# Who issues the stores and weight loads of a Fourier stage: from ScalarE to SP, with two small changes of order

## The reference

```
X = np.fft.rfft(x, axis=1)                       # x: 2 x 3008 x 256
y = np.fft.irfft(X * (filt_r + 1j * filt_i)[None], n=3008, axis=1)
x = y.reshape(6016, 256)
h = x @ w_in;  x = elu(h) @ w_out                # first layer, 256 -> 2048 -> 256
h = x @ w_in2; out = (h * clip(h + 3, 0, 6) / 6) @ w_out2
```

## Time and profile before

| | |
|---|---|
| time, median of 3 | 1148.3 us (1145.12 to 1150.12) |
| time of the profiled execution | 1148.3 us |
| its span | 1145.6 us |
| PE, PEld busy | 1124.9, 1070.5 us |
| DVE, ACT, POOL busy | 850.8, 699.6, 305.0 us |
| Fourier stage | 0 to about 134 us |

### The profile page before, as it was taken

How to read it: one execution, slowest core, us unless ns; L and a number is a source line. 1 busy time by engine, 2 the same in 40 slices (tenths; PEclk the granted TensorE clock), 3 DMA queues, 4 the chain that set the end, 5 groups by cost and what they waited for, 6 DMA issues and landing times.

```text
span 1145.6 us, 17167 instructions
## 1 busy us (share of the span) xinstructions
PE 1124.9 (98%) x6280; PEld 1070.5 (93%) x6280; DVE 850.8 (74%) x1347; ACT 699.6 (61%) x1293; POOL 305.0 (27%) x260
## 2 busy tenths in 40 slices
PE   8999899999999999999998999999999999999998
PEld 4666799999999999999997899999999999999998
DVE  6777388788888888888888876666666666666665
ACT  0222466766666666666666666667666666766665
POOL 4876212030202112121248742120302021121000
PEclk9999999999999999999999999999999999999999
DMA  8886300000000101010021201000000000010000
GB/s 254 270 253 213 102 1 28 29 27 28 28 28 16 39 1 55 1 55 1 28 82 57 91 1 54 1 28 28 27 29 27 28 24 32 1 55 1 28 1 27
DMA packets 33587, 59.50 MB, mean 52 GB/s; under 512 B 3456, under 2 KB 23552, under 8 KB 33504
## 3 DMA queue, kind: packets, MB, share of 16 engines
q1 hardware_dynamic: 27168, 48.06, 13.4%
q10 hardware_dynamic: 6336, 10.36, 2.7%
HBM read 39.92 MB, written 18.48 MB: 51 GB/s over the span
## 4 chain that ended last, share of the span: by engine, by line
PE 91%; DVE 4%; ACT 1%; DMA 1%; issue 1%; POOL 1%; SPq 0%; ACTq 0%
PE ps L360 43%; PE ps L349 13%; PE ps L350 13%; PE ps L351 13%; PE ps L292 2%; PE ps L317 2%; PE ps L308 2%; PE ps L309 2%; DVE e L584 2%; PE ps L300 2%; DVE e L582 1%; DVE g_lo L589 1%; DMA x_ring<-x_dev 1%; ACT e L465 1%; ACT w_hi L442 0%
## 5 line engine op out<-in xcount | busy, mean ns | idle before, releaser
L589 DVE TENSOR_TENSOR g_lo<-e,g_hi 128x376 fp32r<-128x376 f32 (+1 forms) x384 | 285.6, 771 | 113.6 <-ACT g_hi L495 113.3
L349 PE MATMUL ps<-op_hi,w_hi 128*128 128x376 f32 x896 | 300.3, 335 | 0.7 <-DVE h L603 0.7
L350 PE MATMUL ps<-op_hi,w_lo 128*128 128x376 f32 x896 | 299.7, 334 | 0.0
L351 PE MATMUL ps<-op_lo,w_hi 128*128 128x376 f32 x896 | 299.6, 334 | 0.0
L654 POOL TENSOR_TENSOR op_lo<-xr,op_hi 128x752 fp32r<-128x752 f32 x64 | 103.9, 1624 | 623.6 <-ACT op_hi L450 623.6
L360 PE MATMUL ps<-g_hi,w_hi 128*128 128x376 f32 x1024 | 259.1, 334 | 7.3 <-ACT g_hi L495 7.3
L360 PE MATMUL ps<-g_lo,w_hi 128*128 128x376 f32 x1024 | 259.5, 335 | 2.0 <-DVE g_lo L589 1.9
L360 PE MATMUL ps<-g_hi,w_lo 128*128 128x376 f32 x1024 | 259.6, 334 | 0.0
L360 PEld LDWEIGHTS ps<-g_hi,w_hi 128*128 128x128 f32 x1024 | 184.0, 188 | 9.4 <-ACT g_hi L495 9.4
L360 PEld LDWEIGHTS ps<-g_lo,w_hi 128*128 128x128 f32 x1024 | 184.1, 188 | 5.0 <-DVE g_lo L589 5.0
L360 PEld LDWEIGHTS ps<-g_hi,w_lo 128*128 128x128 f32 x1024 | 184.2, 188 | 0.0
(11 more groups left out here) (50 smaller groups left out, 1216.6 us busy)
## 6 DMA issues: line engine op xcount, KB each, us to landing
f_ring<-f_dev SPq DMA_DIRECT2D x32, 384.0 KB, 4.4
xr<-y SPq DMA_DIRECT2D x64, 188.0 KB, 3.0
y<-ystage SPq DMA_DIRECT2D x16, 376.0 KB, 2.5
out_dev<-ystage SPq DMA_DIRECT2D x16, 376.0 KB, 2.5
x_ring<-x_dev SPq DMA_DIRECT2D x15, 384.0 KB, 5.5
y<-ystage ACTq DMA_DIRECT2D x24, 235.0 KB, 2.8
w_raw<-w_dev ACTq DMA_DIRECT2D x16, 256.0 KB, 4.5
w_raw<-w_dev SPq DMA_DIRECT2D x16, 256.0 KB, 2.8
```

The costliest lines, as they stand in the source:

```text
L349: pe.matmul(out, w_hi[:, p, cols], hi, start=start, stop=False, skip_group_check=True)
L350: pe.matmul(out, w_lo[:, p, cols], hi, start=False, stop=False, skip_group_check=True)
L351: pe.matmul(out, w_hi[:, p, cols], lo, start=False, stop=True, skip_group_check=True).then_inc(done, 1)
L589: return dve.tensor_tensor(g_lo[:, tiles, :], e[:, tiles, :], f32(g_hi[:, tiles, :]), ALU.subtract)
```

## The change

SP gets store_piece and all of load_w. In each step it runs load_f, load_x, the store of piece_at(i-1) and, in step w_step(p) - 2, load_w(p); load_w(0) stands behind the first x and filter loads instead of ahead of everything on ScalarE's queue. The last store stands behind the loop, ahead of load_xr(1). On ScalarE the cast weight_hi(p) now stands ahead of the evacuation of its step. The matmul engine runs six warm-up matmuls instead of two. The condition `and i` that goes away changes nothing (at i = 0 the first comparison is false already). The sizes, the slots, the waits and the work of PE, DVE and POOL in each step stay.

```diff
--- before.py
+++ after.py
@@ -219,12 +219,21 @@
                 sp.dma_start(f_ring[:, i % FSLOTS].rearrange("p a n -> p (a n)"),
                              f_dev[c // B, :, g]).then_inc(f_loaded[i % FSLOTS], 16)
 
+            def store_piece(n):
+                pos, j0, nj = piece_cols(n)
+                c = ORDER[pos]
+                at = c % B * S + j0 * ICOL
+                sp.wait_ge(i_evac, n + 1)
+                sp.dma_start(y0[c // B, :, at:at + nj * ICOL],
+                             ystage[:, n % 2, 0:nj * ICOL]).then_inc(y0_stored[n % 2], 16)
+
             def load_w(k):
-                p = k % PAIRS
-                sp.wait_ge(w_lo_done, k - 1)
+                layer, p = k // PAIRS, k % PAIRS
+                if k >= 2:
+                    sp.wait_ge(w_lo_done, k - 1)
                 raw = w_raw[:, k % 2]
-                sp.dma_start(raw[:, 0:4 * P], w_dev[1, p, :, 0:4 * P]).then_inc(w_loaded[k % 2], 16)
-                sp.dma_start(raw[:, 8 * P:12 * P], w_dev[1, p, :, 4 * P:8 * P]).then_inc(w_loaded[k % 2], 16)
+                sp.dma_start(raw[:, 0:4 * P], w_dev[layer, p, :, 0:4 * P]).then_inc(w_loaded[k % 2], 16)
+                sp.dma_start(raw[:, 8 * P:12 * P], w_dev[layer, p, :, 4 * P:8 * P]).then_inc(w_loaded[k % 2], 16)
 
             def load_xr(s):
                 if s:
@@ -258,13 +267,21 @@
             load_f(2)
             load_x(2)
             load_x(3)
+            load_w(0)
             for i in range(NG + PIECES):
-                if FSLOTS <= i + FSLOTS - 1 < NG and i:
+                if FSLOTS <= i + FSLOTS - 1 < NG:
                     load_f(i + FSLOTS - 1)
                 if i % 2 == 0 and XSLOTS <= i // 2 + 3 < NG // 2:
                     load_x(i // 2 + 3)
+                done = piece_at(i - 1)
+                if done is not None:
+                    store_piece(done)
+                for p in range(1, PAIRS):
+                    if i == w_step(p) - 2:
+                        load_w(p)
                 if i == 26:
                     load_xr(0)
+            store_piece(NPIECE - 1)
             for s in range(2 * NS):
                 if s + 1 < 2 * NS:
                     load_xr(s + 1)
@@ -319,7 +336,7 @@
                 last.then_inc(i_done, 1)
 
             pe.wait_ge(zeroed, 1)
-            for _ in range(2):
+            for _ in range(6):
                 pe.matmul(ps[:, 0, :], back[:, 0, 0, :], back[:, 0, 0:4, :].rearrange("p j d -> p (j d)"),
                           start=True, stop=True)
             pe.wait_ge(a_mat_loaded, 16)
@@ -411,28 +428,12 @@
 
         @block.scalar
         def _(act):
-            def store_piece(n):
-                pos, j0, nj = piece_cols(n)
-                c = ORDER[pos]
-                at = c % B * S + j0 * ICOL
-                act.wait_ge(i_evac, n + 1)
-                act.dma_start(y0[c // B, :, at:at + nj * ICOL],
-                             ystage[:, n % 2, 0:nj * ICOL]).then_inc(y0_stored[n % 2], 16)
-
-            def load_w(p):
-                if p >= 2:
-                    act.wait_ge(w_lo_done, p - 1)
-                raw = w_raw[:, p % 2]
-                act.dma_start(raw[:, 0:4 * P], w_dev[0, p, :, 0:4 * P]).then_inc(w_loaded[p % 2], 16)
-                act.dma_start(raw[:, 8 * P:12 * P], w_dev[0, p, :, 4 * P:8 * P]).then_inc(w_loaded[p % 2], 16)
-
             def evac_piece(n):
                 nj = piece_cols(n)[2]
                 act.wait_ge(i_done, n + 1)
                 if n >= 2:
                     act.wait_ge(y0_stored[n % 2], 16 * (n // 2))
                 act.copy(ystage[:, n % 2, 0:nj * ICOL], ps_i(n)[:, 0:nj * ICOL]).then_inc(i_evac, 1)
-                store_piece(n)
 
             def weight_hi(k):
                 p = k % PAIRS
@@ -467,14 +468,12 @@
                     act.activation(dst, src, ACT.Relu, bias=3.0).then_inc(ready, 1)
 
             for i in range(NG + PIECES):
+                for p in range(PAIRS):
+                    if i == w_step(p):
+                        weight_hi(p)
                 n = piece_at(i - 1) if i <= NG else None
                 if n is not None:
                     evac_piece(n)
-                for p in range(PAIRS):
-                    if i == w_step(p) - 2:
-                        load_w(p)
-                    if i == w_step(p):
-                        weight_hi(p)
                 if NG <= i:
                     evac_piece(NPIECE - PIECES + i - NG)
                 if NG - NOP <= i < NG:
```

## The result

The changed kernel takes 1158.26 us (median of 5; 1157.18 to 1158.92) against 1148.9 for the kernel before in the same measurement: a ratio of 1.0084 (95% interval 1.0063 to 1.0103), 9.4 us slower. The forecast was the same 9.4 us, counted from the 1148.3 us of the first three timings: 1157.7 us. Executions of one kernel spread over some 5 us, and part of that is the clock: of the 89 timings of the kernel before that stand beside the experiments, the 21 with a mean granted clock of 1.000 took 1144.7 us on average and the other 68 took 1147.3. The profiled execution of the changed kernel took 1156.32 us with a span of 1154.5, so between the two profiled spans there are 8.9 us to explain.

The account below looks back on a forecast made before the run. The matmul engine, busy 98% of the span, was taken to bound the kernel. Ring 10.9, tail -1.5 and start 0 gave +9.4 on 1148.3, so 1157.7 us, with an 8-in-10 range of 1150.5 to 1164.

Parts of the forecast that it names:

- The ring: Fourier stage: evacuation, store, filter load, sign, sums, cast, back to evacuation; 13.7 us per turn against 11.1, delay 10.9 us.
- four lumps of 2 to 3 us: Fourier stage, 50 to 110 us: idle matmul time, one lump per weight pair, behind DVE's prod_i.
- the formula 5 L: Fourier stage: delay is 5 L - 9.6, L being a filter load from issue to landing, taken as 4.1 us.
- The fixed part of a turn: Fourier stage: one turn without its filter load (store issue, signs, weight_lo, sums, cast, evacuation), put at 9.6 us.
- Entry: Fourier stage, first turn: piece 2's evacuation ends at 50.3 us instead of 46.86.
- the exit: End of the Fourier stage's turns: piece 13 evacuated at 104.9, prod_i(26) at 110.4 instead of 99.52, 10.9 us late.
- The tail: Last output pieces of the Fourier stage: 1.5 us gained; up to 2.0 from the wait, 1.7 more from the clock.
- load_xr(1): Load now behind the last store, some 20 us later: costs nothing, covered by its first ScalarE reader at 159.0.
- The start: Six warm-up matmuls and later first weights at the kernel's beginning: taken as 0 us, ends -0.5 and +1.5.
- rival 1: Fourier stage: unseen slack with filter loads under 3.4 us, so no change within 0.5%; chance 0.20.
- Rival 2: Faster through the last output pieces, 3.7 us off, plus 1.0 at the beginning: 1143.6 us; chance 0.04.
- Rival 3: Fourier stage: clock falls after each turn's 2.6 us idle, at most 6.8 us on top, about 1164 us; chance 0.10.

Follow-up runs that it names:

- 1: The changed kernel with the evacuation ahead of weight_hi again on ScalarE, stores and weight loads still on SP: 1145.84 us, ratio 0.9993 to the kernel before.
- 4: The changed kernel, cast still first, with each store on SP put behind the next step's filter load: 1146.22 us, ratio 0.9999 to the kernel before.
- 2: The kernel before with weight_hi ahead of the evacuation and its store, all stores and weight loads still on ScalarE: 1146.37 us, ratio 1.0003.
- 3: The kernel before with only the stores of y0 moved to SP, the last one behind the loop: 1145.14 us, ratio 0.9987.
- 5: The changed kernel with one more 128x704 subtraction on POOL in weight_lo of pairs 3 to 7: 1164.48 us, ratio 1.0162 to the kernel before.
- 6: The kernel before with one more 128x704 subtraction on POOL in weight_lo of pairs 3 to 7: 1145.25 us, ratio 1.0001.
- experiment 10: The kernel before with six warm-up matmuls instead of two: 1147.93 us, ratio 1.0004.
- 9: The kernel before with one more wait on SP, holding load_xr(1) until the last evacuation, stores still on ScalarE: 1146.3 us, ratio 0.9994.
- 11: The kernel before with only the first layer's weight loads moved to SP, stores on ScalarE, evacuation first: 1147.74 us, ratio 1.0012.

## Why the prediction was right, point by point

**The ring** is shown: its chain stands in the profile, its cost goes away with either of two unlike edits (1 opens it, 4 makes it shorter than PE's own time), it does not exist with either half alone (2 and 3), and work added inside it comes out nearly one for one (5) but is free outside (6). The likeliest case and its mechanism held. One thing stays open. No run has only the cast first and the stores on SP, so what the weight loads on SP and the warm-up add to the ring isn't shown; its chain runs through no weight load after 50 us. And one thing the forecast had only in part: it put all of PE's waits behind prod_i, in four lumps of 2 to 3 us; there were six of up to 1.6 us, and two of them were part_i's own wait for an evacuation, which the forecast didn't name. Both ways end in the same ring, so its length, and not the way, set the time.

**The size of the ring's term** was met (10.9 forecast, 10.4 measured) partly by luck: its errors cancel. The filter load took 4.36 to 4.86 us, 4.63 on average, not 4.1: by the formula 5 L, 2.7 us too little. The fixed part of a turn was 9.3 us (13.67 - 4.36, and 9.29, 9.32, 9.36 for the others), not 9.6: 1.1 too much over four turns. Entry: piece 2's evacuation ended at 50.67, forecast 50.3. So prod_i(26) came at 112.37, 12.9 us late, not 10.9. Then the exit was wrong in kind: I let the ring end with piece 13, but weight_lo(7) still stands ahead of group 27's sign in POOL's program, and prod_i(27) came at 116.60 (103.43 before, in its timeline), 13.2 us late. For PE this exit is worth only 0.3 us: part_r(26) was 10.2 us late, part_r(27) 10.5. And I took DVE's lateness for PE's, which is the largest of the errors beside that of the filter load. In the kernel before, prod_i(27) ended at 103.98 and its first reader, part_r(27), started at 106.67: 2.7 us of slack that the delay uses up first. 13.2 - 2.7 is 10.5.

**The tail** gained 3.3 us where 1.5 was taken. About 2 us are the shorter wait (7.9 us instead of 10.0 between pieces 21 and 27), as bounded by 2.0. The other 1.3 are the clock: the stretch at 0.57 of the earlier trace rows has no counterpart after. That part isn't the change's alone. Experiments 2 and 6 have the kernel before's wait of 4.5 us between pieces and were granted 1.00 throughout the tail, and their first layer started 9.4 us after piece 21's copy, against 10.7 in the kernel before and 7.5 after. My choice of 1.5 was too low by the rows at hand, 2.0 for the wait alone.

**load_xr(1)** was costed at nothing, covered by its first reader at 159.0. That reader indeed did not wait, but the step failed: with the load, POOL's four sums moved out of the tail, where DVE was idle, to DVE's critical first microseconds of the first layer. The main part took 1.5 us more, and of the 1.7 us of experiments 1 and 3 holding the sums back gave 1.1 back. It isn't enough to ask who waits for a moved transfer; the work that it triggers runs beside something else.

**The start** came at +0.3, forecast 0, and experiment 10 agrees. But the profile of the kernel before is a late one. In the seven profiles with two warm-up matmuls part_a(2) began at 10.00 to 11.92 us (its own is the 11.92), in the six with six of them at 11.29 to 12.18. So the longer warm-up may cost a microsecond or so of start in other executions; the timings of experiment 10 don't show it (1.0004, at most 1.0013).

**The rivals.** No filter load in the ring landed under 3.4 us, so rival 1 has its condition against it. Rival 2 stays a mechanism of the tail, worth 3.3 us and less than 0.5%, as said. Rival 3 fell, and without a test: the middle windows show a granted clock of 1.00, but its condition, 2.6 us of idle time at a stretch, never came about, since the longest was 1.6 us. The Trainium skill's rule that transfers run on the same DMA engines whichever engine starts them, and that the choice saves only the issue time ("DMA: Bandwidth & Descriptors", section "Issuing engines are not separate DMA queues") holds where it applies: the medians of experiments 3, 9 and 11 are within 0.2% of the kernel before. It did not give the time of the change, since the cost was in what waits in front of the issue.

## What to carry to other kernels

When a transfer moves to another engine's program, write down for each instruction behind it who waits for it, and follow that until you reach an engine or come back to where you began; a closed ring has a period of its own, and it is free only while that is shorter than what the bounding engine needs for the same steps. Two edits that cost nothing each can close one together, so time them apart and together. Where PE stands idle need not be at the place that you had in mind: follow every wait of the bounding engine into the ring. A store that waits for an evacuation cost nothing behind the next filter load (experiment 4) and, with the cast first, 9.4 us ahead of it.

## What the hardware showed that I had not expected

DVE's work beside POOL's. The changed kernel's timeline at the start of the first layer:

```profile
148.55 1.33 POOL L643 TENSOR_TENSOR xr<-xr 128x376 f32<-128x376 f32 x1 [16.68 <-DMA xr<-y]
148.95 1.15 DVE L581 TENSOR_SCALAR e<-e 128x376 f32<-128x376 f32 x1
...
150.13 0.55 DVE L583 TENSOR_TENSOR e<-ps,e 128x376 f32<-128x376 f32 x1
150.60 2.42 DVE L588 TENSOR_TENSOR g_lo<-e,g_hi 128x752 fp32r<-128x752 f32 x2
150.90 1.71 POOL L646 TENSOR_TENSOR xr<-xr 128x376 f32<-128x376 f32 x1
```

The same two operations in the kernel before, with POOL idle:

```profile
141.57 0.35 DVE L582 TENSOR_SCALAR e<-e 128x376 f32<-128x376 f32 x1
...
142.54 1.40 DVE L589 TENSOR_TENSOR g_lo<-e,g_hi 128x752 fp32r<-128x752 f32 x2
```

0.35 became 1.15 us, 1.40 became 2.42, and POOL's own 0.98 became 1.71, while the tensor_tensor with one input in PSUM stayed at 0.55. The Trainium skill, "SBUF — State Buffer", section "SBUF: two separate sides", says that DVE and GpSimd share one pair of ports, held by one of them for a whole instruction, and that a DVE operation with two SBUF inputs or in a two-port mode needs it. The trace agrees, down to the operation with a PSUM input, which isn't slowed; in which mode the tensor_scalar ran, no row shows.

The clock in the tail: five profiles have PE waiting 1.8 to 2.0 us for an evacuation ahead of piece 25. Three of them were granted a low clock right behind it (0.57 for 3.9 us in the kernel before and about as much in experiment 10, 0.52 for 6.8 us in experiment 11) and two 1.00 (experiments 2 and 6). The eight without that wait were all granted 1.00 in the tail. So a drop that follows a wait in one profile need not be there in the next.
